# Windowed attention on two 64-column tiles: both halves of a step's scores folded into one, two steps at a time

## The reference

```python
scores = np.matmul(q, k.transpose(0, 1, 3, 2)) / np.sqrt(D)      # window = 64
scores = np.where((rel >= 0) & (rel < window), scores, -1e9)     # rel = query - key
attn = np.exp(scores - scores.max(-1, keepdims=True))
attn = attn / (attn.sum(-1, keepdims=True) + 1e-9)
x = np.matmul(attn, v)                    # -> 2304 tokens x 512
h = (x @ w1) * (x @ w2) @ w3 @ w_out      # widths 512, 1024, 1024, 512
h = h @ w_in                              # 512 -> 2048
out = np.maximum(0.01 * h, h) @ w_out2    # 2048 -> 512
```

## Time and profile before

| | before |
|---|---|
| device time, median of 3 | 732.0 us |
| profiled execution: span | 728.8 us (the page gives no other time of it) |
| TensorE matmul busy | 722.2 us, 99% |
| VectorE busy | 530.9 us, 73% |
| ScalarE busy | 416.7 us, 57% |
| GpSimd busy | 101.8 us, 14% |
| first phase, to the first product of 384 columns | about 69.7 us |
| attention ends | about 220 us |
| granted TensorE clock | 1.000 |

### The profile page before, as it was taken

One profiled execution on the slowest core, in us unless ns is written; L12 is line 12 of the kernel. 1 busy time (PEld: TensorE's weight loads), 2 busy tenths in 40 slices (PEclk: granted clock), 3 DMA queues, 4 the chain that ended last, 5 costly groups with the idle time before them and its releaser, 6 DMA issues.

```text
span 728.8 us, 13804 instructions
## 1 busy us (share of the span) xinstructions
PE 722.2 (99%) x5032; PEld 697.9 (96%) x5032; DVE 530.9 (73%) x834; ACT 416.7 (57%) x888; POOL 101.8 (14%) x122
## 2 busy tenths in 40 slices
PE   9999999999999999999999999999999999999998
PEld 7788989999999999999999999999999999999998
DVE  6988888797767679798668968569788655445552
ACT  5876677646664345665555655456677534544541
POOL 3433474413333120000000000000000000000000
PEclk9999999999999999999999999999999999999999
DMA  9884667655754689989857998987996468778773
GB/s 340 291 293 164 206 232 232 200 163 164 244 175 160 195 291 389 324 279 322 289 193 279 318 298 285 364 278 247 381 370 240 128 186 239 206 212 236 208 199 119
DMA packets 96835, 181.13 MB, mean 249 GB/s; under 512 B 7936, under 2 KB 55680, under 8 KB 96768
## 3 DMA queue, kind: packets, MB, share of 16 engines
q1 hardware_dynamic: 90032, 166.62, 69.1%
q10 hardware_dynamic: 6736, 13.63, 5.1%
HBM read 111.80 MB, written 68.42 MB: 247 GB/s over the span
## 4 chain that ended last, share of the span: by engine, by line
PE 61%; DVE 0%; issue 0%; ACT 0%; DVEq 0%
PE acc L406 10%; PE acc L408 9%; PE acc L407 9%; PE ps_pair L406 5%; PE ps_pair L408 5%; PE ps_pair L407 5%; PE ps_more L408 3%; PE ps_values L408 3%; PE ps_more L406 3%; PE ps_values L406 3%; PE ps_more L407 3%; PE ps_values L407 3%; DVE weights_b L1196 0%; DVE arena L1377 0%; DVE arena L1382 0%
## 5 line engine op out<-in xcount | busy, mean ns | idle before, releaser
L406 PE MATMUL acc<-parts,weights_a 128*128 128x384 f32 (+1 forms) x320 | 112.2, 351 | 0.1
L408 PE MATMUL acc<-parts,weights_a 128*128 128x384 f32 (+1 forms) x320 | 109.5, 342 | 0.0
L407 PE MATMUL acc<-parts,weights_a 128*128 128x384 f32 (+1 forms) x320 | 109.3, 341 | 0.0
L406 PE MATMUL acc<-parts,weights_b 128*128 128x384 f32 x320 | 109.1, 341 | 0.2 <-ACT arena L899 0.2
L408 PE MATMUL acc<-parts,weights_b 128*128 128x384 f32 x320 | 107.1, 335 | 0.0
L407 PE MATMUL acc<-parts,weights_b 128*128 128x384 f32 x320 | 107.0, 334 | 0.0
L1462 DVE TENSOR_TENSOR parts<-raw_c,parts 128x768 fp32r<-128x768 f32 x64 | 61.1, 958 | 61.6 <-ACT parts L958 61.5
L958 ACT ACTIVATE parts<-raw_c 128x768 fp32r<-128x768 f32 x64 | 54.0, 846 | 68.9 <-DMA raw_c<-g_between 66.4
L406 PEld LDWEIGHTS acc<-parts,weights_a 128*128 128x128 f32 x320 | 60.1, 188 | 4.6 <-issue 1.7
L841 ACT ACTIVATE arena<-arena,negmax 128x128 f32<-128x128 f32 (+1 forms) x144 | 55.2, 386 | 15.4 <-DVE negmax L1233 15.3
L406 PEld LDWEIGHTS acc<-parts,weights_b 128*128 128x128 f32 x320 | 60.1, 188 | 1.7 <-issue 0.7
(11 more groups left out here) (213 smaller groups left out, 1764.2 us busy)
## 6 DMA issues: line engine op xcount, KB each, us to landing
g_between<-arena SPq DMA_DIRECT2D x75, 384.0 KB, 4.8
raw_c<-g_between SPq DMA_DIRECT2D x64, 384.0 KB, 3.5
arena<-p_between SPq DMA_DIRECT2D x42, 384.0 KB, 5.2
arena<-qk_steps SPq DMA_DIRECT2D x36, 384.0 KB, 5.0
arena<-v_steps SPq DMA_DIRECT2D x36, 256.0 KB, 3.7
p_between<-arena SPq DMA_DIRECT2D x24, 384.0 KB, 5.9
x_between<-arena ACTq DMA_DIRECT2D x21, 384.0 KB, 5.4
arena<-x_between SPq DMA_DIRECT2D x21, 384.0 KB, 5.2
```

Source lines behind the costliest of these rows:

```text
L406: eng.matmul(out_ap, w_hi, m_hi, start=start, stop=False, skip_group_check=resumed)
L407: eng.matmul(out_ap, w_hi, m_lo, start=False, stop=False, skip_group_check=resumed)
L408: return eng.matmul(out_ap, w_lo, m_hi, start=False, stop=stop, skip_group_check=resumed)
```

## The change

Two steps become a pair p = g // 2 (`NDUO` = 18 pairs, `CPAIRS` = 6 in the first phase), and each stage from the mask on works on the pair.

- For query i and key j within 64, exactly one of the two halves is seen: the earlier block where j > i, the own block where j <= i. `fold_copy` (ScalarE) copies the own half of the raw scores to SBUF, and `fold` (VectorE) writes the earlier half over it where the mask says so, by a predicated copy. So `probs` of a pair has 8 x 64 columns, as that of one step had 4 x 128. For a step that opens a batch, constants are written in place of the earlier half.
- The maximum is taken over 512 columns for the pair, then scaled in an instruction of its own (`bias`); the scale of the scores moves into the exponential. 8 exponentials of 64 columns for the pair, in place of 8 of 128.
- Four transposes for the pair, in place of eight. `unfold` (VectorE) reads the turned tiles from PSUM twice, times a 0/1 mask each, to `pt[0]` (earlier keys) and `pt[1]` (own). ScalarE's copies of the turned tiles go.
- `values(p)`: 32 multiplications over 64 keys on 64x64 tiles, in place of 16 over 128 on 128x64 tiles; a step that opens a batch does only its own half. Tiles in the upper and the lower half of the array rows write to different banks (`ps_heads`).
- First phase: scores in slot 2p, transposes in 2p + 3, values in 2p + 4; fold and exponentials in iteration 2p + 1, inversion and normalisation in 2p + 2, unfold in 2p + 4. Second phase: after the scores, fold 1 slot, exponentials 2 and 3, inversion and normalisation 5, transposes and unfold 10, values 12. Scores and values keep their slots.

```diff
+CPAIRS = CSTEPS // 2
+NDUO = NSTEP // 2
+SCORED = {_p: 2 * _p if _p < CPAIRS else slot_of(4 * (_p // CPAIRS - 1), 5 + 6 * (_p % CPAIRS)) for _p in range(NDUO)}
+EXPS_A, EXPS_B, RECIP, TURN, VALUES = 2, 3, 5, 10, 12
+TURNED = {_p: SCORED[_p] + (3 if _p < CPAIRS else TURN) for _p in range(NDUO)}
+VALUED = {_p: SCORED[_p] + (4 if _p < CPAIRS else VALUES) for _p in range(NDUO)}
...
             def load_qk(g):
                 if g >= 2:
-                    sp.wait_ge(scores_done, g - 1)
+                    sp.wait_ge(scores_done, g // 2)
...
+            def fold_copy(p):
+                act.wait_ge(scores_done, p + 1)
+                if p >= 2:
+                    act.wait_ge(turned, p - 1)
+                act.activation(probs[p % 2], ps_own, ACT.Copy).then_inc(fold_copied, 1)
+
+            def exps(p, b):
+                r = p % 2
+                act.wait_ge(bias_done, p + 1)
+                for u in range(b * HP, (b + 1) * HP):
+                    act.activation(probs_flat[r][:, u], probs_flat[r][:, u], ACT.Exp,
+                                   bias=bias[:, r * H + u:r * H + u + 1], scale=float(D) ** -0.5,
+                                   accum_out=sums[:, r * H + u:r * H + u + 1]).then_inc(exp_done, 1)
...
             for k in range(WSLOTS):
-                for g in range(CSTEPS):
-                    if SCORES0[g] + TURN0 == k - 1:
-                        turn_copy(g)
+                for p in range(CPAIRS):
+                    if SCORED[p] == k - 1:
+                        fold_copy(p)
                 for i in pieces_for(k + 1):
                     split_piece(i)
-                for g in range(CSTEPS):
-                    if SCORES0[g] == k - 1:
-                        exps(g, range(HP))
+                for p in range(CPAIRS):
+                    if SCORED[p] == k - 1:
+                        exps(p, 0)
+                        exps(p, 1)
...
+            def fold(p):
+                r = p % 2
+                dve.wait_ge(fold_copied, p + 1)
...
+                if whole:
+                    dve.copy_predicated(probs[r], earlier.unsqueeze(1).unsqueeze(1).to_broadcast([P, 2, HP, BQ]),
+                                        ps_before).then_inc(folded, 2)
...
+                dve.tensor_reduce(negmax[:, rr], probs_flat[r], AX.X, ALU.max, negate=True).then_inc(max_done, 1)
+                dve.wait_ge(max_done, p + 1)
+                dve.tensor_scalar(bias[:, rr], negmax[:, rr], float(D) ** -0.5, None, ALU.mult).then_inc(bias_done, 1)
...
+            def unfold(p):
+                dve.wait_ge(turned, p + 1)
+                if p > 0:
+                    dve.wait_ge(values_done, p)
+                for c in range(2):
+                    dve.tensor_tensor(pt[c].rearrange("p (u q) -> p u q", q=BQ), ps_more.rearrange("p (u q) -> p u q", q=BQ),
+                                      mask_s[:, 1 + c].unsqueeze(1).to_broadcast([P, H, BQ]), ALU.mult).then_inc(unfolded, 1)
...
             for k in range(WSLOTS - 1):
...
+                for p in range(CPAIRS):
+                    if TURNED[p] == k - 1:
+                        unfold(p)
+                    if SCORED[p] == k - 1:
+                        fold(p)
                 if k in P0_LO:
                     split_fill(*P0_LO[k])
...
-                for g in range(CSTEPS):
-                    if SCORES0[g] == k - 1:
-                        invert_sums(g)
+                for p in range(CPAIRS):
+                    if SCORED[p] == k - 2:
+                        invert_sums(p)
...
+                for b in range(2):
+                    for t in range(2):
+                        for c in range(2):
+                            if c == 0 and opens(2 * p + b):
+                                continue
+                            for r in range(2):
+                                for a in range(2):
+                                    d, rows = slice(a * D, (a + 1) * D), slice(r * BQ, (r + 1) * BQ)
+                                    turned_at = ((b * 2 + t) * 2 + (a ^ t)) * BQ
+                                    last = pe.matmul(ps_heads[r][d, t, b], v_raw[rows, b, c, t, a],
+                                                     pt[c][rows, turned_at:turned_at + BQ],
+                                                     start=c == 0 or opens(2 * p + b), stop=c == 1)
```

More of the change, by code:

```diff
@@ L1684, in turn, with values @@
[L1684 to L1701 removed]
+            def values(p):
+                for b in range(2):
+                    pe.wait_ge(v_in[b], 16 * (p + 1))
+                pe.wait_ge(unfolded, 2 * p + 2)
+                pe.wait_ge(x_done, 2 * p)
+                for b in range(2):
+                    for t in range(2):
[9 more added lines that the diff above has]
+                                                     start=c == 0 or opens(2 * p + b), stop=c == 1)
+                last.then_inc(values_done, 1)
@@ new lines, in attention_first @@
+                for p in range(CPAIRS):
+                    if SCORED[p] == k:
+                        scores(p)
+                for p in range(CPAIRS):
+                    if TURNED[p] == k:
+                        turn(p)
+            def attention(n):
+                for p in range(CPAIRS, NDUO):
+                    if VALUED[p] == n:
+                        values(p)
+                for p in range(CPAIRS, NDUO):
+                    if SCORED[p] == n:
+                        scores(p)
```

319 lines of the change are left out of this document (138 added, 181 removed).

## The result

The changed kernel takes 735.2 us (median of four executions; 733.2 to 737.5), the kernel before 732.1 us beside it: ratio 1.0048, 95% interval 1.0025 to 1.0070. In a second set of runs it was 737.1 against 731.7, ratio 1.0073 [1.0056, 1.0090]. It is slower by 0.5 to 0.7 per cent; the forecast was 729.0 us, faster.

A forecast was written before the change was run, and what follows sets the result against it. TensorE, busy in 99% of the span, was taken to bound the kernel. Transposes -7.7, opening steps -0.9, layout -1.4, present waits -2.9, values 0, first phase +5.3, second +4.7 gave -3.0 unrounded: 729.0 us, range 725.5 to 736.5.

The forecast's parts named there:

- rival 1: Predicated copy at the head of the fold costs 1.2 us instead of 0.60: +7.6, 736.5 us, slower; chance 0.20.
- Transposes: On TensorE, 36 groups of four become 18: -5.3 us in the second phase, -2.4 in the first, together -7.7.
- layout: Scores directly after values share 64x64 tiles in 12 places, saving 0.12 us each: -1.4 us.
- opening steps: Four steps that open a batch leave out half their values, 16 records each: -0.9 us.
- values: A values block of 64 records on 64x64 tiles takes 1.08 us, as before: no change.
- Present waits: TensorE's existing waits go: 0.9 us in the first phase, 2.0 around GpSimd's normalisation in the second: -2.9.
- First phase, +5.3 for the new waits: Products late behind fold, splits and exponentials before slots 2, 4, 6, 8, 12: 4.9 us, plus 0.4 for engine contention.
- 0.4 for the times in which GpSimd and VectorE slow each other down: First-phase allowance of 0.4 us for contention, beside 4.9 us of late slots; one split had taken 1.23 instead of 0.68.
- Second phase, +4.7: Copies behind exponentials delay slots 17, 23, 68, 73, 74; late unmasking delays the values of pairs 7 and 8: 4.7 us.
- Time around the span: The median's 3.2 us above the profiled span, 732.0 against 728.8, taken as unchanged: 725.8 span becomes 729.0.
- Rival 4: Queues have less room, delayed products push others, waits larger by half: +2 to +4, 731 to 733 us; chance 0.10.
- Rivals 2 and 3: 2: values tiles work only in pairs, 745 us, chance 0.08. 3: second phase's waits don't appear, 724.3, chance 0.12.

The follow-up runs named there:

- sums_cut: Changed kernel with GpSimd's sums of the first four weight units cut to 16 of their columns; ratio to before 1.0021.
- sums_moved: Changed kernel with GpSimd's sums of the weight units started at other places, when a fold is over; ratio to before 1.0085.
- exps_by_two: Changed kernel with the second phase's eight exponentials of a pair two to a slot in four slots; ratio to before 1.0044.
- values13: Changed kernel with the second phase's values 13 instead of 12 slots behind the scores; ratio to before 1.0086.
- after_warm: Changed kernel with unused identity multiplications where TensorE waits ahead of first-phase slots 2, 4, 6, 8 and 12; 733.7 us, ratio to before 1.0024.
- small_pred: Changed kernel with the predicated copy on 64 of 512 columns; ratio to before 0.9993.
- spread_all: Changed kernel with spread_first and exps_by_two together, and the first weight-sum bank saved ahead of slot 8's exponentials; 729.2 us, ratio to before 0.9968.
- spread_best: spread_all with the second phase's values one slot later (13); 727.9 us, ratio to before 0.9947.
- between: Changed kernel with VectorE's first-phase splits for the next slot between predicated copy and maximum, ScalarE's order unchanged; ratio to before 1.0099.
- pieces_first: Changed kernel, first phase: next slot's first piece split ahead of the fold on ScalarE and VectorE, the second before VectorE's maximum; ratio to before 1.0103.
- spread_first: Changed kernel with the move of between, and a pair's last four first-phase exponentials left to the next slot behind its pieces; ratio to before 1.0004.
- three_moves: Changed kernel with sums_moved, between, and ScalarE's weight-sum banks saved ahead of and between slot 8's exponentials; ratio to before 1.0052.

## Why the prediction was wrong

The forecast was 3.0 us faster, and the kernel is 3.1 us slower or more. 735.2 us lies inside the range of 725.5 to 736.5, which was kept that wide for rival 1, a slow predicated copy; that is not what happened. Slower than before had a chance of 0.29.

- *Transposes, layout, opening steps, values*: right. A group costs 0.35 us and what follows; layout 0.15 for 0.12; 48 records in place of 64 save 0.23 of a block, four times 0.9; the block of 64 takes 1.09 us, 1.08 forecast. The two phases bear the sum out: with their waits taken off, each is as long as laid out.
- *Present waits*: right. GpSimd's is gone.
- *First phase, +5.3 for the new waits*: right in places and mechanism, wrong in size, and this is the step that failed. By starts they are 1.7, 1.4, 1.6, 2.7 and 1.6 us at slots 2, 4, 6, 8 and 12, 9.0 where 4.9 + 0.4 stood (0.6, 1.0, 0.2, 2.3, 0.8). The term "0.4 for the times in which GpSimd and VectorE slow each other down" is 2.5 by sums_cut: I had counted one lengthened split, and it is one at each of the slots 2, 6 and 12 (0.53 us more) and the scaling at 2 and 6 (0.3 and 0.5 more), just where the fold now stands. The sum had 0.72 us from the copy's start to the maximum's; it is 0.79, and adds 0.3 at four slots. VectorE's copy starts 0.84 us (0.77 at slot 2) after the product behind the scores, where the sum had 0.63 for the own scores: 1.0 at five slots. 0.3 us stay open.
- *Second phase, +4.7*: the same failure, right at every place named, too small by 2.0. Slots 17, 23, 68, 73, 74 are late by 1.5, 0.5, 0.8, 0.8, 0.6 (0.5, 0.3, 0.2, 0.6, 0.7), the values of pairs 7 and 8 by 0.8 and 1.2 (1.1, 1.3), two more values by 0.3 each. Slot 17 makes half the difference: the scaling took 0.71 us there too, beside GpSimd's sums, and the copy behind the exponentials came 1.0 later. sums_moved shows the first of these (slot 17's gap 0.7 us with the sums elsewhere), exps_by_two the exponentials ahead of the copies, values13 the late unmasking.
- *What was missing altogether*: the clock. "The granted clock is at its upper level in every slice" was read as a property of the chip; it is one of a kernel whose TensorE hardly stops in its first phase. The forecast put 2.3 us of idleness at slot 8 and priced it at 2.3 us. In five of eight executions the mean clock was 0.998 or less. By after_warm this is at most 1.4 to 3.4 us of the median, of which the late transfer near 390 us may be a part. The miss of 5.6 us in the profiled span has nothing of it: that execution ran at 1.000.
- *Time around the span*: before's profiled span was set against the median, 3.2 us above. The pairs of time and span in later runs have 1.7 to 2.2 us between them; the other 1.2 were spread between executions. With 2.0 the forecast would have been 727.8 and the miss larger.
- *Rivals.* Rival 4 (waits larger by half) is what happened: 15.8 us for 10.0. Its size, +2 to +4, was too low: a later TensorE forgave hardly anything, +5.6 in the profiled span, and with all that moves the medians it is +6 to +8. Rival 1's mechanism is real (small_pred), its price was not. Rivals 2 and 3 fell: a values block took 1.09 us, and the second phase's waits are 6.8 us.

Why the gain can be had all the same: spread_all and spread_best change no amount of work. They take the splits out from behind the fold and halve the bursts of exponentials, and of the 10 us that TensorE saves 2.3 and 3.9 us, by the ratios, appear as time.

## What to carry to other kernels

Folding two steps into one halved the transposes and the normalisations and doubled the burst of exponentials. Where an engine with 75% load (VectorE's in the first phase after) runs level with TensorE, the burst decided, not the load: lay the queue out slot by slot, with GpSimd's instructions beside it, and move what the next product needs in front of the burst or into its middle, on both engines at once: between, which moved VectorE's splits alone, and pieces_first, which put ScalarE's split ahead of its fold copy, made it worse, and spread_first, which moved both, better. Price an idle stretch of TensorE over 2 us at more than its length, and look at several executions' clocks before a median is explained by one profile.

## What the runs showed of the hardware

- A gap of TensorE of 2.2 to 2.8 us is followed, in part of the executions of one kernel, by 6 to 8 products of 512 columns at 0.427 us instead of 0.23. Six kernels whose longest gap was at most 2.0 us (before among them) had no execution at 0.998 or less; a seventh, three_moves, had two of five, with gaps of 1.9 and 2.0 in its one profile.
- With idle products in the gaps the mean clock stayed at 0.999 or more in all nine executions (after_warm).
- Beside a GpSimd addition that reads SBUF, VectorE's scaling of 8 numbers went from 0.17 to 0.71 us and a split of 512 columns from 0.68 to 1.21, while the predicated copy from PSUM (0.76, 0.75 on average) and the maximum (0.69) kept their time. Without the addition the four are 0.17, 0.69, 0.76 and 0.69 (sums_cut).
- 64 values records on 64x64 tiles in 1.09 us, 17 ns each with start and end. The groups behind three prices (line, shapes, count; busy us, mean ns; idle before): the predicated copy, which the trace before could not give, the unmasking, and the normalisation, at the price of the earlier trace rows but half as often:

```profile
L1235 DVE COPY_PREDICATED arena<-arena,ps_pair 128x512 f32<-128x512 int32 x14 | 10.5, 747 | 6.1 <-ACT arena L843 6.1
L1264 DVE TENSOR_TENSOR arena<-ps_values,arena 128x512 f32<-128x512 f32 x36 | 23.0, 680 | 1.9 <-PE ps_values L1721 1.9
L777 POOL TENSOR_TENSOR arena<-arena,rsum 128x512 f32<-128x512 f32 x18 | 21.1, 1174 | 104.5 <-DVE rsum L1257 104.5
```
